# Choosing and loading the first expert before the routing is finished, in a fused attention, MLP and mixture-of-experts kernel

## The chip, the cores and the metric

The kernel runs on one core of one Trainium2 chip. The metric is the device time of one execution in microseconds (us); the time before is 1026.56 us, the median of 3 runs (1025.98 to 1027.63).

## What is computed

The reference chains three stages; all arrays are float32.

```python
for t in range(S):                          # 4 batches, 8 heads, S = 768, D = 48: a decayed linear attention
    S_re, S_im = a[t] * (S_re, S_im) + (k[t] outer v[t], 0);  y[t] = q[t] @ S_re
h = x @ w_in                                # 3072 tokens, 384 -> 2048 -> 384
x = (h * np.tanh(softplus(h))) @ w_out
logits = x @ w_gate + modality_bias[modality_id]     # 8 experts, one of them for each token
e_idx = np.argmax(logits, axis=1)
for e in range(E):
    mask = e_idx == e
    if not mask.any():
        continue
    out[mask] = gate_w[mask, None] * (np.maximum(x[mask] @ w1[e], 0.0) @ w2[e])
```

w1[e] is 384 x 1024 and w2[e] is 1024 x 384, 1.5 MB each.

## The kernel before

Each engine has its own instruction stream, written by hand in one Block; semaphores alone order them.

**Attention and MLP.** The 3072 tokens go through eight slots (m = 0 to 7) of 384 tokens. A slot has 32 gaps g (GAPS), into which TensorE's matmuls of the first MLP layer (`hidden`), of the second (`second`) and of the attention of the slot ahead are woven. The last slot has no attention left. Its second layer is closed by `last_unit`, and ScalarE writes the result to `x2_rows` in HBM. All large products are made of two or three parts (hi and lo parts in fp32r).

**Routing.** VectorE picks each token's expert (`choose`), counts for the first 18 groups of 128 tokens in slot 6 (`count_early`), and places their ranks in slot 7 at g = 22 (`place_ranks`, RANK_AT). After the last slot the same is done for the last 6 groups. The tokens are then sorted by expert in tiles of 128: TensorE sums `order` and the gates into `bank_y` by 24 one-hot products; VectorE copies them out and signals `order_done`. A run is an expert that has tokens, with its number of tiles; the list `runs_i` holds for each run its tiles, its first tile, its expert and the tile from which its weight buffer is free, and VectorE signals `runs_ready`.

**Experts.** TensorE, VectorE and ScalarE loop over the runs and over each run's tiles. There are two buffers of each weight (`w1_sb`, `w2_sb`, taken in turn by `par`). For each tile t, GpSimd gathers 128 rows of `x2_rows` by an indirect DMA (`gather`; `xg`), TensorE turns them (`turn_tokens`), VectorE copies them (`take_tokens`; `xg_t`), TensorE makes 24 products with w1 (48 matmul records in the trace), ScalarE copies `he` out with the ReLU, VectorE splits it, and TensorE makes 24 products with w2. ScalarE scales the result into `o_sb`, and GpSimd scatters it to the output (`scatter`). At the start of a run VectorE splits the run's w2 into `w2_hi` (a cast) and `w2_lo` (a subtraction). SyncE loads w1 and w2 of a run together, once `o_ready` tells that the run before the last is done. `stay_awake(n)` issues n products on TensorE whose result nobody reads. GpSimd copies each tile's column of `order` into `idx_in` ahead of the gather.

## Time and profile before

| | |
|---|---|
| median of 3 runs | 1026.56 us |
| the profiled execution, its own time | 1025.5 us |
| its span in the trace | 1023.7 us |
| TensorE busy | 95% of the span |
| mean granted TensorE clock | 0.986 of full |
| VectorE, ScalarE, GpSimd busy | 70%, 56%, 9% |

The span is what the trace covers; the execution's own time is 1.8 us longer. Of the span about 711 us are attention and MLP (the last matmul of `last_unit` is there), 31 us are the routing's end and the first gather, and the rest is the expert loop: 27 tiles in 4 runs of 13, 2, 1 and 11 tiles. A busy TensorE is no proof of useful work, since the products of `stay_awake` count as busy.

### The profile page before, as it was taken

The page shows a single profiled execution, that of the slowest core. Times are in us where ns is not written, and L with a number is a line of the kernel's source. Part 1 is how long each engine was busy: PE and PEld are TensorE (multiplying, and loading weights), DVE is VectorE, ACT ScalarE, POOL GpSimd, SP SyncE. Part 2 cuts the span into 40 slices and gives each one's busy share as a digit, 9 for nine tenths or more (in the row PEclk, how much of TensorE's full clock was granted, in tenths as well). Part 3 has the DMA queues.
Part 4 walks back from the last instruction along what each step waited for, and adds up shares of the span by engine and source line. Part 5 has one row for each costly group of instructions (what it writes and reads, how often), then busy time and mean ns, then how long its engine had stood idle before and what let it go on. Part 6 is the DMA issues. An engine that isn't in the chain of part 4 may idle for free.

```text
span 1023.7 us, 19054 instructions
## 1 busy us (share of the span) xinstructions
PE 975.4 (95%) x6668; PEld 944.0 (92%) x6669; DVE 711.5 (70%) x1300; ACT 574.0 (56%) x1069; POOL 89.5 (9%) x149
## 2 busy tenths in 40 slices
PE   5889799999999999999999999999799999999996
PEld 3778798999999999999999999999799999999996
DVE  4666998988888988888988877877543333663332
ACT  6557886876777876777778765554022223222221
POOL 2000000000000000000000000000022222442221
PEclk9799999999999999999999999999989999999998
DMA  9702221222222221221131110000341111441110
GB/s 200 229 5 33 40 40 24 40 63 40 40 62 40 40 63 40 40 63 34 31 71 24 24 38 19 1 24 26 115 171 38 46 38 38 159 148 38 38 46 24
DMA packets 146228, 58.66 MB, mean 57 GB/s; under 512 B 131321, under 2 KB 140551, under 8 KB 146160
## 3 DMA queue, kind: packets, MB, share of 16 engines
q1 hardware_dynamic: 139056, 42.61, 17.4%
q0 software_dynamic: 3904, 10.44, 3.2%
q10 hardware_dynamic: 3200, 4.72, 1.2%
q8 instruction: 41, 0.67, 0.3%
q14 instruction: 27, 0.22, 0.1%
HBM read 48.21 MB, written 10.03 MB: 57 GB/s over the span
## 4 chain that ended last, share of the span: by engine, by line
PE 87%; DVE 4%; ACT 4%; issue 2%; DMA 2%; POOL 0%; POOLq 0%; ACTq 0%; SPq 0%; DVEq 0%
PE bank L1650 20%; PE bank L1631 19%; PE bank L1879 14%; PE bank L1890 11%; PE bank L1555 4%; PE bank L1594 4%; PE bank L1542 4%; PE bank L1596 3%; PE bank L1577 3%; PE bank L1496 1%; PE bank L1489 1%; DMA out_dram<-o_sb,idx_out 1%; PE bank L1861 1%; DMA xg<-x_rows,idx_in 1%; PE bank L1620 1%
## 5 line engine op out<-in xcount | busy, mean ns | idle before, releaser
L1879 PE MATMUL bank<-xg_t,w_sb 128*128 128x128 f32 x1296 | 152.2, 278 | 1.9 <-issue 1.6
L1879 PEld LDWEIGHTS bank<-xg_t,w_sb 128*128 128x128 f32 x1296 | 151.3, 195 | 2.4 <-issue 1.9
L1631 PE MATMUL bank<-x_hi,w_in_hi 128*128 128x384 f32 x384 | 141.5, 368 | 1.9 <-DVE x_lo L1089 1.9
L1650 PE MATMUL bank<-w_out_hi,g_hi 128*128 128x392 f32 x378 | 139.0, 368 | 0.0
L1631 PE MATMUL bank<-x_hi,w_in_lo 128*128 128x384 f32 x384 | 130.9, 341 | 0.0
L1631 PE MATMUL bank<-x_lo,w_in_hi 128*128 128x384 f32 x384 | 130.9, 341 | 0.0
L1650 PE MATMUL bank<-w_out_lo,g_hi 128*128 128x392 f32 x378 | 128.6, 340 | 0.0
L1650 PE MATMUL bank<-w_out_hi,g_lo 128*128 128x392 f32 x378 | 128.5, 340 | 0.0
L948 ACT ACTIVATE he<-bank 128x128 f32<-128x128 f32 x216 | 59.7, 277 | 108.4 <-PE bank L1879 105.5
L762 ACT ACTIVATE hid<-bank 128x384 f32<-128x384 f32 x128 | 62.3, 486 | 84.7 <-PE bank L1631 83.9
L952 ACT ACTIVATE o_sb<-bank,gate_now 128x384 f32<-128x384 f32 x27 | 15.7, 581 | 116.1 <-PE bank L1890 111.1
L1631 PEld LDWEIGHTS bank<-x_hi,w_in_hi 128*128 128x128 f32 x384 | 73.2, 191 | 3.6 <-DVE x_lo L1089 2.5
L1890 PE MATMUL bank<-w_hi,he_hi 128*128 128x384 f32 x216 | 74.4, 345 | 0.7 <-DVE he_lo L1461 0.7
L624 POOL COPY idx_in<-order 128x1 int32 (+1 forms) x29 | 7.2, 247 | 772.7 <-issue 667.6
L1631 PEld LDWEIGHTS bank<-x_lo,w_in_hi 128*128 128x128 f32 x384 | 73.3, 191 | 0.8
L1459 DVE CAST he_hi<-he 128x256 fp32r<-128x256 f32 x108 | 31.8, 295 | 60.4 <-ACT he L948 59.7
L1631 PEld LDWEIGHTS bank<-x_hi,w_in_lo 128*128 128x128 f32 x384 | 73.0, 190 | 0.0
L1650 PEld LDWEIGHTS bank<-w_out_hi,g_hi 128*128 128x128 f32 x378 | 71.2, 188 | 1.7
L1650 PEld LDWEIGHTS bank<-w_out_lo,g_hi 128*128 128x128 f32 x378 | 71.2, 188 | 1.6
L1890 PE MATMUL bank<-w_hi,he_lo 128*128 128x384 f32 x216 | 72.3, 335 | 0.0
L1890 PE MATMUL bank<-w_lo,he_hi 128*128 128x384 f32 x216 | 72.2, 334 | 0.0
L1650 PEld LDWEIGHTS bank<-w_out_hi,g_lo 128*128 128x128 f32 x378 | 71.0, 188 | 0.0
(294 smaller groups left out, 2119.9 us busy)
## 6 DMA issues: line engine op xcount, KB each, us to landing
w_sb<-in_moe_w_dram SPq DMA_DIRECT2D x8, 1536.0 KB, 9.3
ab<-in_a_re_dram SPq DMA_DIRECT2D x24, 192.0 KB, 2.9
ab<-in_a_im_dram SPq DMA_DIRECT2D x24, 192.0 KB, 3.3
x_rows<-x_sb ACTq DMA_DIRECT2D x8, 576.0 KB, 3.1
qk_raw<-in_q_dram SPq DMA_DIRECT2D x22, 192.0 KB, 3.3
qk_raw<-in_k_dram SPq DMA_DIRECT2D x22, 192.0 KB, 3.5
v_in<-in_v_dram SPq DMA_DIRECT2D x22, 192.0 KB, 2.8
w_out_sb<-in_moe_w_out_dram SPq DMA_DIRECT2D x4, 768.0 KB, 6.3
```

The lines of the kernel that those rows point to most:

```text
L762: act.activation(hid[:, u % RING, f % QF], bank_h[f % 2][:, 0:TT], ACT.Copy).then_inc(h_copied[f % 2], 1)
L948: act.activation(he[:, f], bank_h[f % 2][:, 0:P], ACT.Relu).then_inc(he_copied[f % 2], 1)
L1459: dve.tensor_copy(he_hi[:, pair], he[:, pair]).then_inc(he_hi_ready, 1)
L1542: last = pe.transpose(t_bank(ch, item)[0:D2, h * C:(h + 1) * C], hat[:, hh, (item // 2) * D2:(item // 2 + 1) * D2], ident[:])
L1555: last = mm((bank_a, bank_b)[j][:, h * C:(h + 1) * C], turned[:, 1, hh], turned[:, 0, hh], start=True, stop=True)
L1577: last = mm(kv_bank(ch)[0:D2, hh * D:(hh + 2) * D], hat[:, hh, D2:], two_heads(vals, hh), start=True, stop=True)
L1594: last = mm(y, weight[:, hh], two_heads(vals, hh), start=True, stop=ch % NC == 0)
L1596: last = mm(y, turned[:, 0, hh], two_heads(state[:, ch % 2], hh), start=False, stop=True)
L1631: last = mm(bank_h[f % 2][:, 0:TT], w[:, kk, f * P:(f + 1) * P], x[:, m % 2, kk], start=(kk == 0 and i == 0), stop=(kk == KD - 1 and i == 2))
L1650: last = mm(bank_x2[t][:, 0:DE], g[:, u % RING, f % QF, t * P:(t + 1) * P], w[:, f], start=(f == 0 and i == 0), stop=(f == FT - 1 and i == 2))
L1879: last = mm(bank_h[f % 2][:, 0:P], w1_sb[par][:, kk, f * P:(f + 1) * P], xg_t[:, kk], start=(kk == 0), stop=(kk == KD - 1))
L1890: last = mm(bank_x2[0][:, 0:DM], h[:, f], w[par][:, f], start=(f == 0 and n == 0), stop=(f == FET - 1 and n == 2))
```

## The change

1. In slot 7, at g = 24, `lead_expert` takes the counts of the first 18 groups (one more small product in `early_ranks`), picks the first expert in the list that has a token there (`lead_i`), and makes a turned order of the experts in which that one stands first (`up_to_e`).
2. SyncE loads that expert's w1 and w2 once the last product of the first MLP layer is done (`h_ready`) and `lead_i` is there. Before, it waited for `runs_ready` and for the end of the MLP.
3. VectorE's list is made in two parts. What the engines need (`runs_i`) comes first; what SyncE needs (`loads_i`) is made by `list_loads` after the first tokens are taken. `order` is written by one instruction that makes integers, ahead of `gate_slot`, and the split of the first run's w2 now stands right behind it, ahead of `take_tokens(0)`.
4. GpSimd's first gather reads `order` itself and no longer waits for a copy of its column or for `runs_i`.
5. For the later runs SyncE loads w2 when the split that read its buffer is done (`w2_lo_ready`), and w1, as before, when the buffer's last run is done.
6. The first run has a loop of its own (without the test for tiles); the pairs of runs start at run 1. `stay_awake` goes from 16, 25, 7 and 22 to 11, 25 and 28.

The core of the diff:

```diff
             sp.wait_ge(slow_known, 1)
-            sp.wait_ge(runs_ready, 1)
-            sp.wait_ge(group_summed, G3)
...
-                    sp.wait_ge(o_ready, at(free))
-                    if par == 1:
-                        sp.wait_ge(gathered, 32)
-                    sp.dma_start(w1_sb[par][:], w1[e].rearrange("(k p) f -> p k f", p=P)).then_inc(w1_in[par], 16)
-                    sp.dma_start(w2_sb[par][:], w2[e].rearrange("(k p) f -> p k f", p=P)).then_inc(w2_in[par], 16)
+            sp.wait_ge(h_ready, NT * FT)
+            sp.wait_ge(lead_ready, 1)
+            leader = sp.value_load(lead_i[0:1, 0:1], min_val=0, max_val=E - 1)
+            w1_load(0, leader)
+            w2_load(0, leader)
+            sp.wait_ge(loads_known, 1)
+            sp.wait_ge(gathered, 32)
+            def next_load(par, run):
...
+                sp.wait_ge(w2_lo_ready, at(split))
+                w2_load(par, e)
+                sp.wait_ge(o_ready, at(free))
+                w1_load(par, e)
+            next_load(1, slice(1, 2))
+            with sp.Fori(0, load_pairs) as i:
+                for par in range(2):
+                    next_load(par, bass.ds(2 * i + 2 + par, 1))
...
-            gather(0)
+            gather_rows(order[:, 0:1])
+            pool.wait_ge(runs_ready, 1)
+            tiles = pool.value_load(runs_i[0:1, TOTALS, 0:1], min_val=1, max_val=MAXT)
...
+            def lead_expert(then, ready):
+                then(dve.tensor_scalar(turn_e[:], bank_a[:, GE * E:(GE + 1) * E], 1.0, None, ALU.min))
+                then(dve.tensor_tensor(turn_e[:], turn_e[:], iota_e[:], ALU.mult))
+                then(dve.tensor_reduce(lead[:], turn_e[:], AX_X, ALU.max))
+                dve.tensor_scalar(lead_i[:], lead[:], -1.0, float(E), ALU.mult, ALU.add).then_inc(ready, 1)
...
-            straight(dve.tensor_copy(gate_slot[:], bank_y[:, GC:2 * GC]))
-            straight(dve.tensor_scalar(order_f[:], bank_y[:, 0:GC], float(N), None, ALU.add))
-            dve.tensor_copy(order[:], order_f[:]).then_inc(order_done, 1)
+            dve.tensor_scalar(order[:], bank_y[:, 0:GC], float(N), None, ALU.add).then_inc(order_done, 1)
+            straight(dve.tensor_copy(gate_slot[:], bank_y[:, GC:2 * GC]))
+            dve.wait_ge(w2_in[0], 16)
+            dve.tensor_copy(w2_hi[0][:], w2_sb[0][:]).then_inc(w2_hi_ready, 1)
+            low_w2(0, 1)
...
             take_tokens(0)
+            list_loads()
...
-            stay_awake(16)
+            stay_awake(11)
             pe.wait_ge(chosen_ready, 2)
...
-            stay_awake(7)
-            pe.wait_ge(order_done, 1)
-            run_pairs = pe.value_load(runs_i[0:1, TOTALS, 1:2], min_val=1, max_val=(E + 1) // 2)
...
-            stay_awake(22)
+            stay_awake(28)
             turn_tokens(0)
+            pe.wait_ge(runs_ready, 1)
+            run_pairs = pe.value_load(runs_i[0:1, TOTALS, 1:2], min_val=1, max_val=E // 2)
+            run_tiles = pe.value_load(runs_i[0:1, RUN_TILES, 0:1], min_val=1, max_val=MAXT)
```

GpSimd's rows around the first gather before (`bank`, `w_sb` and the like are names without their buffer numbers; TENSOR_LOAD and ISA read a number from SBUF into a register):

```order
L601 DMA gl<-ee 8x1x48
L617 TENSOR_LOAD runs_i [waits x2_out,zero_out,order_done]
L617 ISA x2
L624 COPY idx_in<-order 128x1
L627 DMA xg<-x_rows,idx_in 128x384 [waits picked]
L624 COPY idx_in<-order 128x1 [waits xg_turned]
L627 DMA xg<-x_rows,idx_in 128x384 [waits picked]
```

and now:

```order
L622 DMA gl<-ee 8x1x48
L642 DMA xg<-x_rows,order 128x384 [waits order_done,x2_out,zero_out]
L665 TENSOR_LOAD runs_i [waits runs_ready]
L665 ISA x2
L648 COPY idx_in<-order 128x1 [waits xg_turned]
L642 DMA xg<-x_rows,idx_in 128x384 [waits picked]
```

The first gather has moved to the front, reads `order`, and stands ahead of the load of `runs_i`.

VectorE's rows from the end of the list of runs to the first tokens, before:

```order
L1436 CAST runs_i<-runs_f 128x40 [waits dve_own]
L1437 TENSOR_SCALAR runs_i<-runs_i 128x1 [waits dve_own]
L1441 COPY gate_slot<-bank 128x33 [waits order_ready,x2_out]
L1442 TENSOR_SCALAR order_f<-bank 128x33 [waits dve_own]
L1443 CAST order<-order_f 128x33 [waits dve_own]
L1446 TENSOR_LOAD runs_i [waits order_done]
L1446 ISA x2
```

and now (L1482 and L1486 are the split of the first run's w2, L1511 is `take_tokens(0)`, and `list_loads` begins at L1492):

```order
L1473 CAST runs_i<-runs_f 128x27 [waits dve_own]
L1474 TENSOR_SCALAR runs_i<-runs_i 128x1 [waits dve_own]
L1479 TENSOR_SCALAR order<-bank 128x33 [waits order_ready,x2_out]
L1480 COPY gate_slot<-bank 128x33
L1482 CAST w_hi<-w_sb 128x3072 [waits w2_in0,dve_own]
L1486 TENSOR_TENSOR w_lo<-w_sb,w_hi 128x3072 [waits w2_hi_ready]
L1511 COPY xg_t<-bank 128x384 [waits xg_turned]
L1492 TENSOR_SCALAR active<-iota_e 128x8
L1463 TENSOR_TENSOR of_run_x<-of_run,active 128x64 [waits dve_own]
L1465 TENSOR_REDUCE loads_f<-of_run_x 128x8 [waits dve_own]
```

The split of 128 x 3072 elements now stands between `order` and the first tokens; `gate_slot` has moved behind `order`.

TensorE's rows from the last routing product to the turn of the first tile (`xg`), before:

```order
L1852 MATMUL bank<-carried,in_lo 128x66 x11
L1838 MATMUL bank<-earlier,ident 128x128 x7
L1856 TENSOR_LOAD runs_i [waits order_done]
L1856 ISA x2
L1838 MATMUL bank<-earlier,ident 128x128 x22
L1861 MATMUL bank<-ident,xg 128x128 [waits gathered]
L1861 MATMUL bank<-ident,xg 128x128 x2
L1866 UNCONDITIONAL_BRANCH
L1866 ISA
L1869 TENSOR_LOAD runs_i
L1869 ISA x2
```

and now:

```order
L1919 MATMUL bank<-carried,in_lo 128x66 x11
L1905 MATMUL bank<-earlier,ident 128x128 x28
L1924 MATMUL bank<-ident,xg 128x128 [waits gathered]
L1924 MATMUL bank<-ident,xg 128x128 x2
L1951 TENSOR_LOAD runs_i [waits runs_ready]
L1951 ISA x2
L1952 TENSOR_LOAD runs_i
L1952 ISA x2
L1953 UNCONDITIONAL_BRANCH
```

The wait for `order_done` between two groups of unread products is gone, 28 of them stand in one row, and both loads of `runs_i` come behind the turn.

## Rows read from the trace of the kernel before

**Rows 1.** The page's busy times (part 1) and its 40 slices (part 2)

```profile
PE 975.4 (95%) x6668; PEld 944.0 (92%) x6669; DVE 711.5 (70%) x1300; ACT 574.0 (56%) x1069; POOL 89.5 (9%) x149
...
PEclk9799999999999999999999999999989999999998
```

**Rows 2.** Timeline, TensorE, 712 to 751 us

```profile
712.64 3.84 PE L1838 MATMUL bank<-earlier,ident 128*128 128x128 f32 x32 [0.95 <-issue]
...
729.10 1.78 PE L1838 MATMUL bank<-earlier,ident 128*128 128x128 f32 x14
...
740.69 0.55 PE L1861 MATMUL bank<-ident,xg 128*128 128x128 f32 x3 [3.60 <-DMA xg<-x_rows,idx_in]
...
742.87 8.41 PE L1879 MATMUL bank<-xg_t,w_sb 128*128 128x128 f32 x48 [1.64 <-issue]
```

**Rows 3.** Timeline, GpSimd and the SyncE queue, 732 to 746 us

```profile
732.91 0.41 SPq L550 DMA_DIRECT2D w_sb<-in_moe_w_dram  x1
...
733.37 1.11 POOL L627 DMA_INDIRECT xg<-x_rows,idx_in  x1 [0.93 <-POOL idx_in L624]
...
745.99 0.37 SPq L550 DMA_DIRECT2D w_sb<-in_moe_w_dram  x1
```

**Rows 4.** The chain that ended last: start us, us, what

```profile
695.68 1.58 PE bank L1631 x9
...
733.37 7.28 DMA xg<-x_rows,idx_in
...
751.28 0.33 PE bank L1861 x3
```

**Rows 5.** Timeline, VectorE, 698 to 731 us

```profile
698.75 0.56 DVE L1068 TENSOR_SCALAR act_t<-act_t 128x768 f32<-128x768 f32 x1 [1.38 <-ACT act_t L768]
...
727.68 0.17 DVE L1425 TENSOR_SCALAR active<-iota_e 128x8 f32<-128x8 f32 x1
...
728.91 0.22 DVE L1427 TENSOR_TENSOR of_run_x<-of_run,active 128x64 f32<-128x64 f32 x1
...
729.55 0.17 DVE L1431 COPY runs_f<-runs_f 128x7 f32<-128x7 f32 x1
...
730.56 0.19 DVE L1441 COPY gate_slot<-bank 128x33 f32<-128x33 f32 x1
...
731.02 0.18 DVE L1443 CAST order<-order_f 128x33 int32<-128x33 f32 x1
```

**Rows 6.** Windows of 1 us: busy, clock, share of DMA, GB/s

```profile
742.00:743.00 1.00, 0.13 (x1) 0.14 (x1) 0.00 (x0) 0.00 (x0) 0.65 (x1) 0.50 1.06 373
```

**Rows 7.** Timeline of all engines at the last two changes of expert

```profile
892.14 1.76 DVE L1472 CAST w_hi<-w_sb 128x3072 fp32r<-128x3072 f32 x1 [1.27 <-issue]
...
893.93 3.36 DVE L1474 TENSOR_TENSOR w_lo<-w_sb,w_hi 128x3072 fp32r<-128x3072 f32 x1
...
895.19 3.01 POOL L637 DMA_INDIRECT out_dram<-o_sb,idx_out  x1 [1.25 <-ACT o_sb L952]
...
904.41 0.58 ACT L952 ACTIVATE o_sb<-bank,gate_now 128x384 f32<-128x384 f32 x1 [5.01 <-POOLq L651]
...
904.94 1.76 DVE L1472 CAST w_hi<-w_sb 128x3072 fp32r<-128x3072 f32 x1 [4.22 <-DMA w_sb<-in_moe_w_dram]
...
905.84 1.77 POOL L627 DMA_INDIRECT xg<-x_rows,idx_in  x1 [0.84 <-POOL idx_in L624]
...
909.68 0.55 PE L1861 MATMUL bank<-ident,xg 128*128 128x128 f32 x3 [0.19 <-DMA xg<-x_rows,idx_in]
...
910.96 0.41 PE L1890 MATMUL bank<-w_hi,he_hi 128*128 128x384 f32 x1 [0.73 <-DVE he_lo L1461]
```

**Rows 8.** The chain, 889 to 920 us

```profile
889.56 4.18 PE bank L1890 x24
...
915.36 5.36 PE bank L1879 x48
```

**Rows 9.** DMA issues of the page (part 6): KB each, us to landing

```profile
w_sb<-in_moe_w_dram SPq DMA_DIRECT2D x8, 1536.0 KB, 9.3
```

More of the change, by code:

```diff
@@ L1154, in slot @@
                         count_early(straight, chosen_ready)
+                    if m == NT - 1 and g == LEAD_AT:
+                        lead_expert(straight, lead_ready)
                     if m == NT - 1 and g == RANK_AT:
@@ L1238, in slow_route @@
                 place_ranks(then, bank_a, 0, GE)
+                lead_expert(then, s_led)
                 dve.wait_ge(s_exped_all, 1)
@@ L1464, in _ @@
             take_tokens(0)
+            list_loads()
+            dve.wait_ge(runs_ready, 1)
+            run_pairs = dve.value_load(runs_i[0:1, TOTALS, 1:2], min_val=1, max_val=E // 2)
+            run_tiles = dve.value_load(runs_i[0:1, RUN_TILES, 0:1], min_val=1, max_val=MAXT)
+            with dve.Fori(0, run_tiles) as j:
+                expert_tile(j)
             with dve.Fori(0, run_pairs) as i:
-                for par in range(2):
-                    run = bass.ds(2 * i + par, 1)
+                for par in (1, 0):
+                    run = bass.ds(2 * i + 2 - par, 1)
                     run_tiles = dve.value_load(runs_i[0:1, RUN_TILES, run], min_val=0, max_val=MAXT)
@@ L1862, in turn_tokens, with expert_tile @@
                 last.then_inc(xg_turned, 1)
[L1864 to L1865 removed]
+            def expert_tile(par, loaded, nth, t):
+                pe.wait_ge(w1_in[par], loaded)
+                pe.wait_ge(xg_copied, at(t + 1))
+                for f in range(FET):
+                    pe.wait_ge(he_copied[f % 2], at(FET // 2 * t + f // 2))
+                    for kk in range(KD):
+                        last = mm(bank_h[f % 2][:, 0:P], w1_sb[par][:, kk, f * P:(f + 1) * P], xg_t[:, kk],
+                                  start=(kk == 0), stop=(kk == KD - 1))
+                    last.then_inc(he_ready, 1)
+                turn_tokens(t + 1)
+                pe.wait_ge(o_copied, at(t))
+                pe.wait_ge(w2_hi_ready, nth)
+                pe.wait_ge(w2_lo_ready, at(nth))
+                for f in range(FET):
+                    pe.wait_ge(he_hi_ready, FC * t + f // 2 + 1)
+                    pe.wait_ge(he_lo_ready, FC * t + f // 2 + 1)
+                    for n, (h, w) in enumerate(((he_hi, w2_hi), (he_hi, w2_lo), (he_lo, w2_hi))):
+                        last = mm(bank_x2[0][:, 0:DM], h[:, f], w[par][:, f], start=(f == 0 and n == 0),
+                                  stop=(f == FET - 1 and n == 2))
+                last.then_inc(o_ready, 1)
+            stay_awake(28)
+            turn_tokens(0)
+            pe.wait_ge(runs_ready, 1)
+            run_pairs = pe.value_load(runs_i[0:1, TOTALS, 1:2], min_val=1, max_val=E // 2)
+            run_tiles = pe.value_load(runs_i[0:1, RUN_TILES, 0:1], min_val=1, max_val=MAXT)
+            with pe.Fori(0, run_tiles) as j:
+                expert_tile(0, 16, 1, j)
             with pe.Fori(0, run_pairs) as i:
[L1867 to L1868 removed]
+                for par in (1, 0):
+                    run = bass.ds(2 * i + 2 - par, 1)
                     run_tiles = pe.value_load(runs_i[0:1, RUN_TILES, run], min_val=0, max_val=MAXT)
```

139 lines of the change are left out of this document (74 added, 65 removed).

## The prediction

> **What bounds the kernel now.** I read the page first. TensorE is busy for 95% of the span, and its granted clock is full in all slices but one in the last third [rows 1]. So TensorE's stream is the bound, and time can be won where it waits, where it runs unread products, and where its clock is low. The timeline around 740 us shows all three: `stay_awake` fills the time of the routing, then TensorE waits 3.60 us for the first gather, and after a further pause of 1.64 us its first 48 matmuls of the expert loop take 8.41 us [rows 2]. The same 48 take 5.36 us further on [rows 8]. The windows say why: at 742 us the granted clock is 0.50, which is 1.2 of 2.4 GHz [rows 6]. The low clock costs 3.05 us.
>
> The chain of waits says who made TensorE wait: the first gather, issued at 733.37, landed 7.28 us later [rows 4]. Its instruction was done at 734.48, so 6.2 us went by in the transfer, while the loads of w1 and w2 had been on the queue since 732.91 [rows 3]. A gather beside no load is in rows 7: its instruction ended at 907.61, and TensorE, which waited for it, went on at 909.68, so 2.1 us.
>
> A second loss is at the last change of expert. Steady work is 5.36 + 0.33 + 4.18 = 9.87 us a tile [rows 4, 8]. From 893.74 (end of the second layer's 24 products) to 915.36 are 21.62 us for two tiles; 19.74 were needed. 1.9 us are lost, because w2 of the last run landed only at 904.94, its split ended near 910.1, and the products that need it began at 910.96 [rows 7, 8]. ScalarE too was late there: `o_sb` had to wait until 904.41 for a scatter that ran beside both loads [rows 7].
>
> **The change part by part.** All times are on the clock of the trace of before.
>
> *Slot 7.* The added small product is two matmul records of 0.12 us (3.84 us for 32) [rows 2]: everything behind it comes 0.24 us later. `lead_expert` adds eight small VectorE instructions at about 0.2 us [rows 5], 1.7 us. They hold back the work on `hid`, and VectorE had 1.38 us of idle time before 698.75 [rows 5], with more behind. I take nothing for it; if it reached TensorE through g_lo, it would cost up to 1.7.
>
> *The first loads.* The last product of the first layer ends at 697.3 [rows 4]. The two loads go out then, take about 9 us [rows 9], and are there by 708, with nothing else on the queues. The split of w2 (1.76 + 3.36 us [rows 7]) leaves the loop and moves ahead of the first tokens.
>
> *The list and `order`.* In front of `order_done` VectorE loses L1425 (0.2), the two instructions from 728.91 (0.5), the copy at 729.55 (0.2) and two of the three from 730.56 to 731.20 (0.45) [rows 5]. `order_done` comes at 731.20 + 0.24 - 1.35 = 730.1.
>
> *The gather.* Between a signal and GpSimd's indirect DMA stand 0.84 to 0.93 us [rows 3, 7]; I take 0.9, since the wait is of the same kind, with 0 as the lower bound. It starts at 731.0. But VectorE has begun the cast of w2 at about 730.35, and it ends at 732.1. Rows 7 show what that does. The scatter issued at 895.19, during the subtraction of 893.93 to 897.29, took 3.01 us and ended 0.91 after it. The gather issued at 905.84, during the cast of 904.94 to 906.70, ended at 907.61, again 0.91 after, though the next subtraction had begun at once. So I expect the end at 733.0 and, with 2.1 us, the rows at 735.1, not at 740.65. With no delay at all it would be 733.3.
>
> *The unread products.* They start at 729.10 + 0.24, and 28 of them at 0.24 us [rows 2] last until 736.1. That is 1.0 us behind the gather: the fillers, not the gather, now decide, and the uncertainty of the gather is covered as long as it lands by 736.1. The first 11 instead of 16 end 1.2 us earlier, and TensorE waits there for VectorE anyway; I take nothing.
>
> *The start of the loop.* Before, the first matmul came 2.18 us after the first turn (740.69 to 742.87 [rows 2]), with two loads of `runs_i` and two loop heads in between. Now there are two loads and one loop head. VectorE's pair of loads with its heads cost 1.27 us [rows 7]; with the turn's 0.55 that is 1.82. I take 2.0, within 1.8 to 2.2. The matmuls begin at 738.1. TensorE's longest pause is then about 1.5 us, and the clock should stay full: 5.36 us, end at 743.5. Before, the end was 742.87 + 8.41 = 751.28. **Gain 7.8 us.**
>
> *What lies beside it.* `list_loads` is 15 VectorE instructions, 3.0 us, behind the first tokens (737.2), plus 1.3 us for its loads: free at 741.5. The first pair of `he` splits (a twelfth of the w2 split's 5.1 us and its fixed costs, under 1 us) is there by 742.5, and TensorE wants it at 743.8. Cover 1.3 us. SyncE's next loads wait for the second gather and leave at about 743, now three in a row: w2 and w1 of run 1, then w2 of run 2, since its buffer is free. They overlap the gather of tile 2 (issued near 745.1). With the 6.2 us of the loaded gather it lands at 752.3; TensorE wants it at 743.5 + 0.33 + 4.18 + 5.36 = 753.4. Cover 1.1 us.
>
> *Later changes of expert.* w2 of the last run is now asked for when the split of run 1 is done, some 15 us earlier, and only w1 stays at 893.9. The split no longer waits, and the scatter has half the traffic beside it. The 1.9 us should go. **Gain 1.9 us.** At the change before, w1 and w2 are sent 3 us apart instead of together; the traffic is the same, and I take nothing.
>
> *Sum.* 7.8 + 1.9 = 9.7 us. The profiled execution took 1025.5 us for a span of 1023.7, and its median neighbour 1026.56, so the execution is 1.1 below the median. 1026.56 - 9.7 = 1016.9 (span near 1014.0).
>
> **A rule that speaks against it.** In the trace GpSimd's DMA instruction gets through between the cast and the subtraction, and then costs 0.91 us more [rows 7]; the sum goes by that. The Trainium skill, "SBUF — State Buffer", "Who interferes with whom", says that VectorE and GpSimd share a port pair by an exclusive lock, and that the second to issue blocks until the first is done; "SBUF: two separate sides" there adds that GpSimd then cannot write a DMA's descriptors. The trace agrees for one instruction. Read as a bar on the gather for as long as VectorE has such instructions, it gives the second rival.
>
> **The rivals.**
>
> *(a) As forecast*, 1016.9 (own range 1015.9 to 1018.0): 60%.
>
> *(b) The gather is held for the whole split.* Cast and subtraction end at 735.5; 0.91 and 2.1 later, at 738.5, the rows are there, 2.4 us behind the fillers. 1019.3. For it: the scatter that met a subtraction ended only after it. Against: the one that met a cast passed the seam. If the pause also lowers the clock, 3.05 more, 1022.4. 15%.
>
> *(c) The three loads in a row, or the eight instructions in slot 7, cost what they leave little cover for*: the gather of tile 2 or the first scatter lands 1 to 3 us late, or the last change of expert keeps its 1.9 us. 1018.0 to 1020. For it: covers of 1.1 to 1.3 us, and 7.28 us for a gather beside loads. 14%.
>
> *(d) The clock falls in the routing*, because 11 products in place of 16 make the pause ahead of the late ranks 1.2 us longer, soon after one of 0.95 us [rows 2]. 25 fillers and 24 routing products then run at half speed until it is back; 25 x 0.24 = 6.0 us more for the fillers at the most: 1022.9. For it: the fall at 742 came after two pauses. Against: those were 3.60 and 1.64 us long. 6%.
>
> *(e) w2 of the first run is late, and the time gets worse.* VectorE now waits for it before it takes the first tokens. If SyncE's loads did not leave before the list is known, they would land near 745, as before; tokens would wait for the split, and the first matmuls would begin at about 745 + 5.1 + 1.6 (as from the turn's end at 741.24 to 742.87 [rows 2]) = 751.7 at the low clock, 8.8 us behind those of before. With the 1.9 us that is 1033.5. It costs from a landing at about 731 on, and turns the sum into a loss from about 738. Against it: `h_ready` and `lead_i` are there 33 us earlier. 3%. The case that it lands near 738, or that the change doesn't load early what it should and loses what it wins elsewhere, within 2 us of before: 2%.
>
> **How the numbers follow.** The predicted time is (a)'s. To leave out no more than 2 in 10, the range reaches over (c) and the better part of (b), up to 1020.5; at the lower end the gain could be 0.7 larger if the loop starts 0.2 us sooner and the fillers, the scatters and both changes of expert give a little more: 1015.4. A measurement of this kernel can tell 0.2%, 2.05 us, from no change. Faster: (a) to (d), 95%, of which I keep 94%; same 3%; slower 3%.
>
> **What the profile after would show.** The loads at 698 us; the first DMA_INDIRECT near 731, about 2 us long if it met the cast; the cast and subtraction from 730.3 to 735.5; 56 records of fillers in one piece up to 736.1 and no wait for `xg` behind them (a wait means (b)); the first 48 matmuls near 738.1 in 5.36 us at clock 1.00; `w_hi` of the last run without a wait for a DMA, and two tiles there in 19.7 us. The prediction is wrong if TensorE waits more than 1 us for `xg` at tile 0 or 2, if the clock is low anywhere from 715 to 750, or if slot 7 ends more than 0.5 us later than before.

## The result, and the profile after

The changed kernel takes 1014.43 us (median of 4 runs, 1013.44 to 1015.71), the kernel before 1026.71 beside it (1025.98 to 1027.63). The ratio is 0.9886, 95% interval 0.9871 to 0.9900: 10.3 to 13.2 us faster, 11.7 in the middle. The forecast was 9.7 us, with a range up to 11.2. The direction and the mechanism of the gather came out; the size is outside the range (1014.43 is below 1015.4), because two terms of the sum were wrong. The profiled execution took 1014.67 us for a span of 1012.9.

The page's busy times and slices, to be laid beside [rows 1]:

```profile
PE 971.2 (96%) x6658; PEld 940.5 (93%) x6659; DVE 714.6 (71%) x1317; ACT 574.0 (57%) x1069; POOL 90.1 (9%) x148
...
PEclk9799999999999999999999999999999999999998
```

TensorE runs fewer unread products, and the slice with a low clock around 740 us is gone (the low digits of the first two slices and the last one are there in both). The timeline of TensorE from the end of the MLP, beside [rows 2]:

```profile
714.09 2.72 PE L1905 MATMUL bank<-earlier,ident 128*128 128x128 f32 x22 [1.27 <-issue]
...
716.78 0.42 PE L1911 MATMUL bank<-chosen,earlier 128*128 128x48 f32 x2
...
729.10 6.47 PE L1905 MATMUL bank<-earlier,ident 128*128 128x128 f32 x56
...
735.40 0.49 PE L1924 MATMUL bank<-ident,xg 128*128 128x128 f32 x3
...
736.63 5.62 PE L1933 MATMUL bank<-xg_t,w_sb 128*128 128x128 f32 x48 [0.74 <-DVE xg_t L1511]
```

There is no wait for `xg` ahead of the turn at 735.40 (3.60 us before), the first 48 products begin 1.23 us behind the turn's start, and take 5.62 us, not 8.41. Rows of VectorE, GpSimd and SyncE's queue, beside [rows 3, 5]:

```profile
699.19 0.41 SPq L546 DMA_DIRECT2D w_sb<-in_moe_w_dram  x1
...
743.09 0.43 SPq L546 DMA_DIRECT2D w_sb<-in_moe_w_dram  x1
...
729.65 0.19 DVE L1479 TENSOR_SCALAR order<-bank 128x33 int32<-128x33 f32 x1
...
729.97 1.76 DVE L1482 CAST w_hi<-w_sb 128x3072 fp32r<-128x3072 f32 x1
730.77 1.93 POOL L642 DMA_INDIRECT xg<-x_rows,order  x1 [665.24 <-DVE order L1479]
731.77 3.36 DVE L1486 TENSOR_TENSOR w_lo<-w_sb,w_hi 128x3072 fp32r<-128x3072 f32 x1
```

The first loads leave at 699.19. `order` is done at 729.84. The gather starts 0.93 us later in the middle of the cast, and ends at 732.70, 0.97 us behind the cast, while the subtraction had begun at 731.77. The chain at the last change of expert, beside [rows 8] and the rows of [rows 7]:

```profile
894.54 5.50 PE bank L1933 x48
900.05 0.33 PE bank L1924 x3
900.38 4.17 PE bank L1944 x24
904.54 5.36 PE bank L1933 x48
```

Two tiles there take 19.86 us (894.54 to 914.40). Before they took 21.62.

**Where the 11.7 us are.** The last product of the MLP ends at 711.69 us before and at 712.82 after, each on its own clock. In the profiled executions of this study that point lies anywhere from 710.1 to 717.2 us. Almost all of that spread arises ahead of slot 7's rank products, where the kernels do all but the same work: from the first of these products (650.14; 651.05 after) to the end of the MLP it is 61.55 or 61.56 us in all eight traces of the kernel before and its variants, and 61.77 or 61.78 in all of the changed kernel and its variants but after_slot8 (62.03). So slot 7 costs 0.22 us. The rest is counted from the end of the MLP. From there to the last product of the kernel it is 302.22 us before (1013.91) and 290.27 after (1003.09), 11.95 less. The rank products of slot 7, before and after:

```profile
650.14 0.41 PE L1716 MATMUL bank<-chosen,earlier 128*128 128x144 f32 x2
...
651.05 0.41 PE L1783 MATMUL bank<-chosen,earlier 128*128 128x144 f32 x2
```

The parts of the gain, in us:

| stretch | before | after | gain | forecast |
|---|---|---|---|---|
| slot 7, first rank product to the end of the MLP | 61.55 | 61.77 | -0.22 | -0.24 |
| end of the MLP to the last batch of fillers (729.10 on both clocks) | 17.41 | 16.28 | 1.13 | 0 |
| from there to the first product of the second layer (751.61; 742.58 in the chain) | 22.51 | 13.48 | 9.03 | 8.04 |
| last change of expert, two tiles | 21.62 | 19.86 | 1.76 | 1.9 |

Together that is 11.7 us, against a forecast of 9.7. (Its 7.8 us are the first three lines: 8.04 less the 0.24 of slot 7.) Two things were missed: 1.1 us in a stretch that the sum left at nothing, and 1.0 us at the start of the loop. Fillers, here and below, are the unread products of `stay_awake`, two records each.

### The profile page after: what moved, and what is told of

Read it like the earlier page. It is cut to its first block, busy times and chain, and to the rows that moved or that the text cites. A ratio compares the mean times of both kernels' runs of the same rounds, so it can differ in the third digit from the quotient of the medians.

```text
span 1012.9 us, 19018 instructions
## 1 busy us (share of the span) xinstructions
PE 971.2 (96%) x6658; PEld 940.5 (93%) x6659; DVE 714.6 (71%) x1317; ACT 574.0 (57%) x1069; POOL 90.1 (9%) x148
## 4 chain that ended last, share of the span: by engine, by line
PE 90%; ACT 4%; DVE 3%; issue 2%; DMA 0%; POOL 0%; SPq 0%; ACTq 0%; DVEq 0%; POOLq 0%
PE bank L1717 20%; PE bank L1698 19%; PE bank L1933 14%; PE bank L1944 11%; PE bank L1622 4%; PE bank L1661 4%; PE bank L1609 4%; PE bank L1663 3%; PE bank L1644 3%; PE bank L1556 1%; PE bank L1563 1%; PE bank L1924 1%; PE bank L1905 1%; PE bank L1687 1%; PE bank L1747 1%
## 5 line engine op out<-in xcount | busy, mean ns | idle before, releaser
L1933 PE MATMUL bank<-xg_t,w_sb 128*128 128x128 f32 x1296 | 149.2, 275 | 0.7 <-DVE xg_t L1511 0.7
L1933 PEld LDWEIGHTS bank<-xg_t,w_sb 128*128 128x128 f32 x1296 | 148.4, 192 | 1.2 <-issue 1.2
L795 ACT ACTIVATE act_t<-act_t,ratio_bias 128x768 f32<-128x768 f32 x64 | 59.5, 930 | 15.9 <-DVE hid L1095 15.9
```

The source lines that it names most:

```text
L795: act.activation(act_t[:, u % 2], act_t[:, u % 2], ACT.Ln, scale=1.0 / CENTRE, bias=ratio_bias[:, 0:1]).then_inc(ln_ready, 1)
L1933: last = mm(bank_h[f % 2][:, 0:P], w1_sb[par][:, kk, f * P:(f + 1) * P], xg_t[:, kk], start=(kk == 0), stop=(kk == KD - 1))
```

## The experiments

Ratios are to the kernel before, run beside each.

### The start of the loop: fillers, reads and the clock

The forecast let 2.0 us go by between the turn and the first product, for two reads of `runs_i` and a loop head. Theory A: TensorE's sequencer, which issues its instructions and reads numbers into registers, runs ahead and does the reads while fillers are still queued, so that they cost nothing as long as the queue is full. Rival: they stand in line behind the turn.

```diff
 after_fill34:            -stay_awake(28)  +stay_awake(34)
 after_fill20:            -stay_awake(28)  +stay_awake(20)
 after_fill26:            -stay_awake(28)  +stay_awake(26)
 after_two_reads and after_fill34_two_reads, ahead of run_tiles:
+            for _ in range(2):
+                pe.value_load(runs_i[0:1, TOTALS, 1:2], min_val=1, max_val=E // 2)
```

> The changed kernel with 34 unread products in place of 28: six more at 0.23 us, 1.4 us. All theories: the turn is 1.4 us later, at 736.8, and the first matmuls at 738.0; the time is 1.4 us above the changed kernel. It is the base for the run with two more reads.

> 34 unread products and two more reads of a number of the list on TensorE behind the first turn (their values are not used), 0.65 us each. Theory A: the sequencer passes the turn at 734.8 and makes all four reads while the queue still holds products, so the first matmuls begin at 738.0 as with 34 products alone. Theory B: 1.3 us later, at 739.3.

> The changed kernel (28 unread products) with two more reads of the list on TensorE behind the first turn, 0.65 us each. Theory A: the sequencer is ready at 736.4 with two reads, just when the first tokens are copied, so two more show nearly in full: first matmuls at 737.8, 1.2 us later. Theory B: 1.3 us later, too.

> The changed kernel with 20 unread products in place of 28 ahead of the first turn; they end near 733.7, 1.9 us sooner. Theory A (TensorE's sequencer reads the list while its queue still holds unread products, so the pause behind the turn is hidden only as long as they last): the turn is at about 734.7, when the gather lands, but the reads take about 1.9 us from there and the first matmuls begin at 736.5 to 736.9 as in the changed kernel, no gain. Theory B (the pause behind the turn is 1.2 us in the new code, whatever stands ahead): they begin at 735.9, 0.7 us sooner. Theory C (the forecast: products decide, pause 2.0 us) would give 736.7 too, but then the changed kernel should have begun at 737.4.

> The changed kernel with 26 filler products instead of 28 before the turn of tile 0. Fillers decide when the turn starts and the gather has landed by 734.8 us, so the turn starts 0.4 to 0.46 us earlier. If the clock stays full, the time is 1014.0, ratio 0.9996 to the changed kernel (not to be told from it by time, only in the trace); if it falls as it did with 20 fillers, the first 48 products take 7.2 us and the time is 1015.6.

Times in the last two columns are us in the profiled execution.

| kernel | median us | ratio (interval) | fillers' start to first product | the 48 products |
|---|---|---|---|---|
| changed | 1014.43 | 0.9886 (0.9871 to 0.9900) | 7.53 | 5.62 |
| after_fill34 | 1015.37 | 0.9904 (0.9889 to 0.9919) | 8.88 | 5.62 |
| after_fill34_two_reads | 1016.15 | 0.9912 (0.9896 to 0.9929) | 8.99 | 5.62 |
| after_two_reads | 1016.99 | 0.9919 (0.9904 to 0.9933) | 8.84 | 7.25 |
| after_fill20 | 1015.55 | 0.9894 (0.9879 to 0.9908) | 7.44 | 7.24 |
| after_fill26 | 1014.64 | 0.9880 (0.9863 to 0.9896) | 7.43 | 5.62 |

Two more reads cost 1.31 us behind 28 fillers and 0.11 us behind 34. That is theory A. The trace's records of TensorE's sequencer (`--source` of the two lines that read) show it directly. The turn's products start at 735.40 in the changed kernel and at 736.51 in after_fill34. The reads stand behind them in the stream. In the changed kernel:

```profile
L1951 PEldq TENSOR_LOAD <-runs_i x1: 315/315/315, 734.8 to 734.8; - x1
L1952 PEldq TENSOR_LOAD <-runs_i x1: 306/306/306, 735.5 to 735.5; - x1
```

and in after_fill34:

```profile
L1951 PEldq TENSOR_LOAD <-runs_i x1: 317/317/317, 734.9 to 734.9; - x1
```

There the first read comes 1.6 us ahead of the turn's products. So the sequencer passes the turn once the gather has landed and starts on the reads, whatever products are still queued; in the changed kernel the gather had landed by 734.8, 2.1 us after its instruction. Two lower bounds follow for the first product, both worked out from these traces: the turn's start + 1.23 us (changed and after_fill34), and the landing + 1.7 to 1.8 us for two reads and the heads, + 0.65 for each read more. The second is read where TensorE waited for the gather: 1.71 us behind the turn's start in after_fill20 and after_gather_copy. In the changed kernel the bounds give 736.6 and 736.5 to 736.6. after_two_reads: its gather's instruction ended at 731.38, so 731.38 + 2.1 + 1.8 + 1.3 = 736.6 (measured 736.59). after_fill26 by the same sum 740.9 to 741.0 (measured 740.90), and by the fillers 740.6: the reads are last there. In the kernel before the loop began 2.2 us behind the landing; its sequencer read at 740.9 and after, and its 1.64 us of idle time without a releaser cover these reads and the heads.

Timeline of TensorE in after_fill20, and the window of 738 to 740 us (busy time of each engine, granted clock, DMA share, GB/s):

```profile
734.73 0.55 PE L1924 MATMUL bank<-ident,xg 128*128 128x128 f32 x3 [1.05 <-DMA xg<-x_rows,order]
...
736.44 7.24 PE L1933 MATMUL bank<-xg_t,w_sb 128*128 128x128 f32 x48 [1.17 <-DVE xg_t L1511]
...
738.00:740.00 2.00, 2.00 (x12) 2.00 (x12) 0.82 (x6) 0.56 (x2) 0.00 (x0) 0.54 0.37 107
```

Eight fillers fewer (1.80 us) bring the turn only 0.6 us forward, as it now waits for the gather, and the clock falls: 0.54 in that window, near the lower of its two levels (1.2 of 2.4 GHz). TensorE had only stood for 1.05 us ahead of the turn and 1.17 us behind it. after_two_reads stood for 2.04 us at one go and lost the clock too (its 48 products took 7.25 us). The changed kernel stands for 0.74 us and keeps it. With 26 fillers it is 7.43 us instead of 7.53, too little to tell in the ratio. So 28 fillers are near the best number, by the trace; the ratios of 20, 26, 28 and 34 overlap.

before_fill39 asks what the clock alone is worth in the kernel before:

```diff
-            stay_awake(22)
+            stay_awake(39)
```

> The kernel before with 39 unread products in place of 22 ahead of the first turn, so that TensorE has work until the gather lands at about 740.7 us; nothing else is changed. If the low clock alone costs 3.05 us there, the first 48 matmuls take 5.4 us in place of 8.4, they begin at about 742.9 as before, and the time is 3.0 us below before (1023.7). If the clock is not what makes them slow (a rival: w1 or the copies come late), they stay at 8.4 us and the time is that of before.

1027.69 us, ratio 1.0012 (1.0000 to 1.0024), where 3.0 us less had been expected: a miss. Its timeline of VectorE and TensorE:

```profile
743.57 5.62 PE L1879 MATMUL bank<-xg_t,w_sb 128*128 128x128 f32 x48 [1.74 <-issue]
...
745.93 1.76 DVE L1472 CAST w_hi<-w_sb 128x3072 fp32r<-128x3072 f32 x1 [3.50 <-DMA w_sb<-in_moe_w_dram]
...
747.72 3.36 DVE L1474 TENSOR_TENSOR w_lo<-w_sb,w_hi 128x3072 fp32r<-128x3072 f32 x1
...
751.95 0.41 PE L1890 MATMUL bank<-w_hi,he_hi 128*128 128x384 f32 x1 [2.44 <-DVE he_lo L1461]
```

The clock stayed full and the 48 products took 5.62 us instead of 8.41, but the second layer began at 751.95, since the split of w2 ended only at 751.08. Counted from the end of the MLP that is 39.66 us, and it is 39.67 in the kernel before: two things held the same place. Then TensorE, having stood for 2.44 us, lost the clock in the second layer instead (two windows, columns as above):

```profile
752.00:754.00 2.00, 2.00 (x9) 2.00 (x10) 1.90 (x7) 0.00 (x0) 1.16 (x2) 0.74 1.04 388
754.00:756.00 2.00, 2.00 (x8) 2.00 (x7) 0.26 (x1) 0.00 (x0) 0.00 (x0) 0.50 1.07 376
```

From the MLP's end to its last product this kernel needs 303.63 us, 1.4 more than before. The low clock's 3.05 us could be had only because the changed kernel also took the split away from there.

### The early load of w2, the gather and the split

```diff
 after_first_late (SyncE; the first loads wait for the list, as before)
-            sp.wait_ge(h_ready, NT * FT)
+            sp.wait_ge(runs_ready, 1)
+            sp.wait_ge(group_summed, G3)
             sp.wait_ge(lead_ready, 1)
 after_gather_copy (GpSimd)
+            tiles = pool.value_load(runs_i[0:1, TOTALS, 0:1], min_val=1, max_val=MAXT)
...
-                pool.wait_ge(picked, t)
+                pool.wait_ge(picked, t + 1)
...
-            gather_rows(order[:, 0:1])
-            pool.wait_ge(runs_ready, 1)
-            tiles = pool.value_load(runs_i[0:1, TOTALS, 0:1], min_val=1, max_val=MAXT)
+            gather(0)
 after_split_behind (VectorE)
-            dve.wait_ge(w2_in[0], 16)
-            dve.tensor_copy(w2_hi[0][:], w2_sb[0][:]).then_inc(w2_hi_ready, 1)
...
-            low_w2(0, 1)
...
             take_tokens(0)
+            dve.wait_ge(w2_in[0], 16)
+            dve.tensor_copy(w2_hi[0][:], w2_sb[0][:]).then_inc(w2_hi_ready, 1)
+            low_w2(0, 1)
             list_loads()
 after_w2_with_w1 (SyncE)
-                sp.wait_ge(w2_lo_ready, at(split))
-                w2_load(par, e)
                 sp.wait_ge(o_ready, at(free))
                 w1_load(par, e)
+                w2_load(par, e)
```

> The changed kernel, but the first expert's w1 and w2 are loaded only once the list of runs is known and the MLP is summed, as before. By the forecast's case (e): w2 lands near 745, VectorE splits it ahead of the first tokens, TensorE begins at 751 to 752 at the low clock and the time is near 1033, 17 to 19 us above the changed kernel and above the kernel before. If the early load is worth only what the gather gains by an empty queue, the time is 4 to 6 us above the changed kernel.

1028.01 us, ratio 1.0017 (1.0006 to 1.0028). Timeline:

```profile
736.15 0.55 PE L1925 MATMUL bank<-ident,xg 128*128 128x128 f32 x3 [1.69 <-DMA xg<-x_rows,order]
...
740.73 1.76 DVE L1483 CAST w_hi<-w_sb 128x3072 fp32r<-128x3072 f32 x1 [11.89 <-DMA w_sb<-in_moe_w_dram]
...
746.49 8.18 PE L1934 MATMUL bank<-xg_t,w_sb 128*128 128x128 f32 x48 [9.79 <-DVE xg_t L1512]
```

The loads left at 729.41, w2 landed at 740.73, and the tokens stood behind the split: the loop began at 746.49, at a low clock. This is rival (e)'s mechanism. w2 landed 4 us sooner than the forecast had it for this case, so the loss against the kernel before is small. Against the changed kernel it is 13.6 us (17 to 19 had been expected): with the split ahead of the first tokens, nothing is gained unless the load is early. What the other parts would be worth with a late load and the split in its old place no run shows.

> The changed kernel, but the first gather waits for a read of the list and for its column's copy, as before (about 2.1 us from the signal in place of 0.8). The copy or the gather then meets VectorE's split: the gather's instruction ends 0.9 us after the cast or after the subtraction. If it ends after the subtraction (735.1), rows land near 738, TensorE waits 2.5 us, and the time is 3 to 4 us above the changed kernel. If it slips through at the seam, nothing changes, since the unread products cover it.

1019.35 us, ratio 0.9933 (0.9919 to 0.9947). Timeline of GpSimd and TensorE:

```profile
730.63 0.93 POOL L650 COPY idx_in<-order 128x1 int32<-128x1 int32 x1 [665.34 <-DVE order L1479]
...
732.49 3.40 POOL L644 DMA_INDIRECT xg<-x_rows,idx_in  x1 [0.93 <-POOL idx_in L650]
...
738.02 0.55 PE L1924 MATMUL bank<-ident,xg 128*128 128x128 f32 x3 [2.68 <-DMA xg<-x_rows,idx_in]
...
739.73 7.00 PE L1933 MATMUL bank<-xg_t,w_sb 128*128 128x128 f32 x48 [1.17 <-DVE xg_t L1511]
```

The copy came in the middle of the cast and took 0.93 us instead of 0.18, up to the cast's end, and so the gather's instruction missed the seam between cast and subtraction. It lasted from 732.49 to 735.89, 0.98 us beyond the subtraction, and the clock fell (7.00 us for the 48 products). This is rival (b), at 4.9 us, forecast at 2.4 without and 5.5 with the clock; the expectation for this run, 3 to 4 us, was too low because it left the clock out. That the gather reads `order` itself, with no copy and no read of the list ahead of it, is worth those 4.9 us, and not the 0.2 us of a copy: it gets GpSimd to the seam in time.

> The changed kernel with the split of the first run's w2 (cast and subtraction) moved behind take_tokens(0) on VectorE. The first gather then meets no locking instruction: it should take 1.0 us as in the kernel before and end near 731.1 instead of 732.7, and its rows land near 733.2, but the 28 fillers decide the turn's start, so nothing is gained. The split ends near 741.7, 0.9 us ahead of the first second-layer product at 742.6, so it costs nothing either; the list of later loads ends 5 us later, which could cost up to 1 us at the first change of expert. Theory A (covers hold): 1014.4 to 1015.5, ratio 0.9886 to 0.9900. Rival: the second layer waits for the subtraction, 1016 to 1018.

1021.40 us, ratio 0.9951 (0.9937 to 0.9964): a miss by 6 us. Timeline:

```profile
730.57 1.10 POOL L642 DMA_INDIRECT xg<-x_rows,order  x1 [665.21 <-DVE order L1479]
...
738.05 3.36 DVE L1484 TENSOR_TENSOR w_lo<-w_sb,w_hi 128x3072 fp32r<-128x3072 f32 x1
...
744.26 0.15 DVE L1502 TENSOR_SCALAR loads_i<-loads_i 128x1 int32<-128x1 int32 x1
...
745.82 0.15 DVE L1511 COPY gate_now<-gate_slot 128x1 f32 x1 [1.41 <-issue]
...
746.92 0.66 PE L1943 MATMUL bank<-w_hi,he_hi 128*128 128x384 f32 x1 [4.48 <-DVE he_lo L1518]
```

The gather took 1.10 us, undisturbed, and gained nothing under the fillers, as expected. But I had looked only at the product that needs `w_lo`. Behind the subtraction stood `list_loads`, the reads of `runs_i` and the loop heads; the first split of `he` came at 746.02, and TensorE stood for 4.48 us and lost the clock over it (0.50 from 748 to 752 us).

> The changed kernel, but w2 of the later runs is loaded together with w1, once the run before the last is done, as before. By the forecast w2 of the last run lands some 11 us after its issue, its split and a scatter beside the loads are late, and 1.8 to 1.9 us come back at the last change of expert: 1.8 us above the changed kernel. If part 5 of the change is worth nothing, the two are equal within 0.3 us in the trace.

1016.20 us, ratio 0.9903 (0.9888 to 0.9918). The chain at the last change of expert:

```profile
884.52 10.53 DMA w_sb<-in_moe_w_dram
...
897.40 2.74 issue
...
901.10 4.40 PE bank L1943 x24
905.50 5.36 PE bank L1932 x48
```

From the end of the tile before (883.89) to 905.50 two tiles took 21.61 us, as before, and this kernel needs 1.79 us more than the changed one from the MLP's end to its last product. The gain at the last change comes from w2's earlier load, as forecast.

### The 1.1 us behind the MLP

In the kernel before, VectorE's first instruction of `choose` started 1.78 us after the end of the MLP, though ScalarE's last copy, for which it waits, was over at 712.28; the row names no releaser. In the changed kernel it starts 0.63 us after, right behind ScalarE. Between `low_places` and `choose` lies only the read of a flag and the branch over VectorE's slow path, which is never entered. Theory J: how long the jump takes depends on where the code lies. Rival K: the work executed in slot 7 shortens it. Six kernels were made to tell, all with memsets of one column (before_slot7 and before_skip7 were timed in 12 runs each, the other four in one each: slot2 1026.05 us, slot15 1025.61, slot7_g2 1025.59, after_slot8 1014.54, with one run of the kernel before beside them at 1028.65):

```diff
 before_slot7, before_slot2, before_slot15 (7, 2, 15 of them), after_slot8 (8); before_slot7_g2: g == 2
+                    if m == NT - 1 and g == 24:
+                        for _ in range(7):
+                            straight(dve.memset(best[:, 0:1], 0.0))
 before_skip7 (in slow_route, never executed)
+                for _ in range(7):
+                    then(dve.memset(best[:, 0:1], 0.0))
```

> The kernel before with 7 more small instructions inside VectorE's slow branch, which is never executed: only the place of the code behind the branch moves, as it moves in the changed kernel. Theory J (where the code behind the branch lies sets how long VectorE needs after jumping it): the first instruction of choose() starts within 0.1 us of the end of ScalarE's last copy of the MLP, as in the changed kernel, instead of 1.2 us behind it, and the time falls by about 1.1 us, to 0.9990 of before. Rival K (the jump itself costs the same whatever lies behind; something executed earlier in the changed kernel, such as the instructions in slot 7, is what shortens it): VectorE still idles 3.8 to 3.9 us with no releaser, time as before.

> The kernel before with 7 small memsets executed on VectorE in slot 7, group 24, where the changed kernel calls lead_expert. They move the branch and all behind it by 7 instructions, and the branch keeps its length. Theory J, if the place of the target alone matters: as with 7 more in the branch, a start within 0.1 us of ScalarE's copy, 0.9990 of before. Theory J, if it is the distance between branch and target: no change, 1.000. Rival K (work executed in slot 7 shortens it): gain here and none with the instructions inside the branch.

> The kernel before with the 7 small memsets of VectorE at group 2 of slot 7 instead of group 24. Place of the code (theory J): from the end of the MLP's last product to the first instruction of choose() 0.6 us, as with the 7 at group 24, since the branch lies at the same place. Work shortly before the branch (theory K): 1.8 us, as in the kernel before.

> The kernel before with 2 memsets on VectorE at group 24 of slot 7. Theory J: 0.6 or 1.8 us, whichever the new place gives, nothing between or another fixed value. Theory K: near 1.8 us, a little less than without.

> The kernel before with 15 memsets on VectorE at group 24 of slot 7. Theory J: either value, by the place. Theory K (more work before it, shorter): 0.6 us or less.

> The changed kernel with 8 memsets more on VectorE at group 24 of slot 7. Theory J: either value, and if the place matters in steps of 16 instructions or less, the longer one, 1.8 us, is possible here. Theory K: 0.6 us, never more than in the changed kernel.

VectorE's branch in the kernel before (`--source L1371`) and its timeline in before_skip7:

```profile
L1371 DVEq COMPARE_BRANCH  x1: 72/72/72, 710.5 to 710.5; - x1
...
711.94 0.21 DVE L1182 TENSOR_TENSOR biased<-logits,bias_all 128x48 f32<-128x48 f32 x1 [4.00 <-issue]
```

The branch and the timeline in after_slot8, and the timeline in before_slot7_g2:

```profile
L1410 DVEq COMPARE_BRANCH  x1: 72/72/72, 712.7 to 712.7; - x1
...
713.46 0.21 DVE L1208 TENSOR_TENSOR biased<-logits,bias_all 128x48 f32<-128x48 f32 x1 [1.68 <-ACT x_sb L808]
...
712.43 0.21 DVE L1185 TENSOR_TENSOR biased<-logits,bias_all 128x48 f32<-128x48 f32 x1 [2.79 <-ACT x_sb L785]
```

| | before | skip7 | slot2 | slot7 | slot7_g2 | slot15 | changed | after_slot8 |
|---|---|---|---|---|---|---|---|---|
| MLP's end to `choose`, us | 1.78 | 1.83 | 1.77 | 0.63 | 0.62 | 0.62 | 0.63 | 0.63 |

The pause belongs to the jump. From the branch's start (713.47 is the first instruction in the kernel before, whose branch is at 710.5) it is 3.0 us before, in skip7 and in slot2, and 2.8 in before_fill39. In the short cases `choose` waits for ScalarE, so only an upper bound is seen: 0.8 us in after_slot8. The jump itself differs by at least 2 us; 1.15 of them show behind the MLP.

What shortens it is less settled. Seven or fifteen instructions ahead of the branch make it short, two do not, and at which place in slot 7 the seven run makes no difference, which speaks against work done shortly before the branch. Seven in the part jumped over do not shorten it, against what I expected of J in its first form (that the place behind the branch alone matters). The rest fits J, if it is the place of the branch that counts, in steps. But in every short case at least seven more instructions were also executed, and no kernel was run with instructions ahead of the branch that are never executed; so J is argued and K in its widest form stands. How the engine fetches its code no run here shows.

The short jump alone changes nothing in the total: before_slot7 took 1027.74 us, ratio 1.0004 (0.9991 to 1.0017), and before_slot7_g2 needs 302.22 us from the MLP's end to its last product, as before. (before_skip7, with the long jump, took 1027.38 us, ratio 1.0010, 0.9999 to 1.0022.) At the late ranks it gives only 0.31 us (their first product 4.81 us behind the MLP, not 5.12), because TensorE's 32 filler records are then last there; the changed kernel has 22. And what is left at the gather, which leaves 0.4 us sooner, is lost in its transfer beside the loads: 6.77 us from the end of its instruction to the turn, instead of 6.21.

```diff
 after_awake16:          -stay_awake(11)  +stay_awake(16)
 before_slot7_awake11:   before_slot7_g2 and  -stay_awake(16)  +stay_awake(11)
```

> The changed kernel with 16 filler products instead of 11 between the MLP and the late ranks, as in the kernel before. Theory L (with the jump short, the fillers are last there, and the 11 are worth something): the late ranks' first product starts 4.8 to 5.0 us after the end of the MLP instead of 3.96, and all behind it comes 0.8 to 1.0 us later; 1015.3, ratio near 0.9895. The forecast's step (TensorE waits there for VectorE anyway, the 11 are worth nothing): 3.96, no change.

> The kernel before with the 7 memsets of VectorE in slot 7, group 2, which make the jump short, and with 11 filler products instead of 16. Theory L: late ranks' first product 4.0 us after the end of the MLP instead of 5.12 (and 4.81 with 16), order_done 1.1 us earlier against the end of the MLP. In the total nothing or up to 0.5 us, since in this kernel the gather and its loads move along but land no earlier (they did not with the 7 alone) and the clock is low: ratio 0.9995 to 1.0005. Forecast's step: 4.8 as with 16.

| kernel | median us | ratio (interval) | MLP's end to late ranks | to the last product |
|---|---|---|---|---|
| before | 1026.71 | | 5.12 | 302.22 |
| before_slot7_g2 | 1025.59 (one run) | | 4.81 | 302.22 |
| before_slot7_awake11 | 1023.68 | 0.9982 (0.9969 to 0.9995) | 3.97 | 300.58 |
| after_awake16 | 1016.14 | 0.9909 (0.9893 to 0.9924) | 4.53 | 291.62 |
| changed | 1014.43 | 0.9886 (0.9871 to 0.9900) | 3.96 | 290.27 |

TensorE's timeline in before_slot7_awake11:

```profile
712.28 2.72 PE L1841 MATMUL bank<-earlier,ident 128*128 128x128 f32 x22 [0.88 <-issue]
715.37 0.42 PE L1847 MATMUL bank<-chosen,earlier 128*128 128x48 f32 x2 [0.36 <-DVE late_run L1198]
```

Together, the short jump and 11 fillers make the kernel before faster by 1.6 us in the trace and 1.8 (0.5 to 3.2) by the ratio, more than the 0.5 that I allowed. 1.15 us of them are there at the late ranks; besides, this gather needed 5.74 us from its instruction to the turn, and why it was quicker no run shows. The changed kernel loses 1.35 us with 16 again. At the late ranks it is 0.57 us, less than the 0.8 to 1.0 expected, since the fillers started 0.41 us sooner behind the MLP than in the changed kernel (that pause lies between 0.85 and 1.4 us in these traces), and 0.44 us are left at the last batch of fillers. The rest comes at the turn: its gather's instruction ended at 732.82 and the rows came 3.1 us later, not 2.1, so that TensorE waited 0.25 us, and the first product came 1.80 us behind the turn instead of 1.23. Why the rows took longer there no run shows; the 1.80 us are theory A's, counted from the landing.

## Why the prediction was right, and where it was wrong

**The gather and the unread products: right.** The last batch of fillers starts at 729.10; the forecast had it at 729.34. Counted from there the gather starts after 1.67 us (forecast 1.66), its instruction ends after 3.60 (3.66), 0.97 us behind the cast (0.91), and its rows are there after at most 5.7 (5.76). The rows of a scatter and a gather some 170 us further on carried over to the tenth. The fillers decide the turn, as forecast. The gather's instruction took 1.10 us with no split beside it (after_split_behind), 1.93 with the cast and 3.40 with the subtraction (after_gather_copy). The Trainium skill ("SBUF — State Buffer", "Who interferes with whom") states an exclusive lock on the port pair that VectorE and GpSimd share, under which the later instruction blocks; the traces agree.

**Slot 7: right,** 0.22 for 0.24, and `lead_expert` cost TensorE nothing (the cover is thin: the eight memsets more of after_slot8 cost 0.25 us there). The forecast named as a sign of being wrong that slot 7 ends more than 0.5 us later than before. On the clock of the trace it ends 1.13 later, but 0.9 of this is there when its rank products start.

**The start of the loop: the failed step.** "Now there are two loads and one loop head [...] I take 2.0, within 1.8 to 2.2." Measured 1.23. The row that priced it, VectorE's pair of loads at 1.27 us, is of an engine that has nothing queued while it reads. TensorE here reads ahead, under queued products, from the landing of the gather on. With the forecast's own times that would have been 737.3 (736.1 + 1.23; 735.1 + 1.8 is less) and not 738.1. I had hung the reads on the turn, and they hang on the gather. That is 0.8 of the 1.0 us. Besides, the 28 fillers lasted 6.30 us, not 6.72 (the 0.12 us a record came from the 3.84 us of a batch of 32, which include the last product's own length; in the batch of 56 it is 0.113 from start to start), and the 48 products 5.62, not 5.36.

**The 11 fillers in place of 16: the second failed step.** "TensorE waits there for VectorE anyway; I take nothing." It was right for the trace of before, and wrong behind the change, where the jump ahead of `choose` is short and VectorE is no longer late. Measured 1.13 us for jump and fillers together, and 1.15 in before_slot7_awake11. The one does almost nothing without the other: 0.31 us for the jump alone; and in the kernel before TensorE waits 0.33 us for VectorE ahead of the late ranks, so that fewer fillers alone could give nothing (no kernel was run for that).

**The low clock.** The forecast booked 3.05 us to the clock. The full clock is there, but before_fill39 shows that the low clock was one of two causes for the same microseconds, with w2's split the other.

**The last change of expert: right,** 1.76 for 1.9, and gone again in after_w2_with_w1. **`lead_expert` and `list_loads` hidden: right** in the profiled execution; no wait of TensorE above 0.74 us is left from 720 to 760. Rival (c) showed itself once, in after_fill34_two_reads, whose four tiles around two changes of expert took 41.05 us instead of 39.4 beside a scatter that needed 8.10 us. **Rivals (b) and (e)** have the mechanisms forecast; (b) cost 4.9 us, between its two prices, and (e) cost less than forecast, at a landing 4 us sooner. **(d)** did not come: the granted clock is 1.00 in every window of 10 us from 700 to 760.

**The lower end of the range** was not its own sum: a gain larger by 0.7 gives 1016.2, and for the further 0.8 us down to 1015.4 the forecast names no term.

**The profiled execution against the median.** I took the one of before as 1.1 us below its median. The stretches give 11.7 us and so do the medians, so this adds nothing to the miss; that they agree to the tenth is luck, since the interval reaches from 10.3 to 13.2.

## What to carry to other kernels

Count TensorE's register reads from the moment its sequencer comes free (the last semaphore it waited for), and not from the end of the work ahead of them: under queued products two reads cost 0.11 us here, behind a drained queue 1.31 us and the clock. Work taken off an engine that waits is worth nothing only as long as it waits: ask what else the change does to the engine waited for. And before a loss is booked to one cause, ask what ends at the same place a moment later: w2's split stood right behind the low clock. Moving a piece of work further back on an engine holds up everything that stood behind its new place too, as after_split_behind did.

## What the hardware showed that I had not expected

- VectorE's jump over the same skipped code took 3.0 us from the branch to the next instruction in some kernels and at most 0.8 us in others that differ by a few instructions ahead of it.
- The clock fell after pauses of 1.05 and 1.17 us with 0.55 us of work between them, and after one of 2.04; it held after one of 0.74, after 0.25 and 1.26, after one of 1.08 (after_fill26), and in before_fill39 after one of 1.74, but fell there after one of 2.44.
- GpSimd's DMA instruction gets through a seam of 0.03 to 0.04 us between the cast and the subtraction, if it is there in time, and ends 0.91 to 0.98 us later; otherwise it is held for the whole of the subtraction.
